# When the weights are loaded beside the tiles of attention: one by one with every third tile

## The chip, the cores and the metric

The kernel runs on one core of a Trainium2 chip. The metric is the device time of one execution in microseconds (us), as a median over several runs. It is written for the engines directly: TensorE (PE) for matmuls, VectorE (DVE), ScalarE (ACT), GpSimd (POOL), and SyncE (SP), whose queue issues all the DMAs of the kernel. The engines meet by semaphores alone.

## The reference

Three networks in a row, all in float32.

```
# attention with decay, batch 8, heads 8, sequence 576, head width 64
scores = (q @ k.T) / sqrt(64)
ret    = scores * gamma[h] ** (i - j)   where i >= j, else 0
x      = ret @ v                        # -> 4608 tokens x 512
# soft mixture of experts, 8 experts x 4 slots
logits = x @ phi                        # 4608 x 32
d = softmax over tokens(logits);  c = softmax over slots(logits)
slot_in = d.T @ x;  slot_out[e] = relu(slot_in[e] @ w1[e]) @ w2[e]
x = c @ slot_out
# product of two linear maps
h = ((x @ fw1) * (x @ fw2)) @ w3;  out = h @ w_out
```

## The kernel before

**Attention** goes over 36 tiles (NTILES, four groups of nine). A tile is 128 rows of q, k and v for all eight heads, 1 MB, and its rows are two chunks of 64 of the recurrent form of the attention. `load_tile` (L439 to L444) brings tile n into `pkg_sb`, which has four places (SLOTS_IN). From tile 4 on it first waits for `out_ready`, that is until TensorE has used tile n - 4 for the last time. The first two tiles come in two halves each (`load_first`). GpSimd scales the V of each tile by a decay (`scale_v`, L561) as soon as the tile has landed; TensorE may touch the tile's scores only after that.

On TensorE, `step` (L741 to L769) handles tile n: it begins with the scores and state updates of tile n + 1 (`scores`, L648, and `update`, L661, which wait for the scaled V), then takes the logits of tile n - 2 (L711), the part of the output that goes through the states (L676), the part through the scores, first half (L693), the transpose of tile n - 1 (`turn_x`, L705), and the second half (L693), at whose end `out_ready` is counted up. In three of the steps a `dispatch` (L727, L732) is added. The steps stand in a hardware loop over four tiles (L777 to L779, nine passes), so the instructions of the first pass are run again in the other eight. VectorE masks the scores (L1207), sums the states (L1230) and scales the output (L1249); ScalarE copies it (L1007).

**Weights.** There are 36 expert units of 1 MB (`unit_a`, `unit_x` and others: w1, w2, fw1 and fw2) and six fold parts of 1 MB (`fold_raw`: w3 twice and w_out, two parts each, called by g = 0, 1, 2 and j = 0, 1). `load_first_unit` (L452) loads the units 0 to 5, which have places of their own, during attention, with one semaphore `first_units_loaded`. `load_fold` (L446) loads the fold parts; four of them, (0, 0), (2, 0), (0, 1), (2, 1), come during attention. Every load is one `dma_start` in SyncE's program, and SyncE waits at a semaphore in its own order. So a load stands in the queue where the program puts it: unit 0 behind tile 3; the units 1 and 2 behind tile 4; 3 and 4 behind tile 5; 5 behind tile 8; the fold parts behind the tiles 10, 11, 14 and 15 (FOLD_AT). From tile 16 on only tiles are loaded.

Who uses them: ScalarE splits the fold parts into a high and a low piece (`split_hi`, L1052 to L1066), three times during attention, at the tiles 18, 22 and 26 (FOLD_HI_AT, the first four rows of j = 0 serve the first four splits), the rest behind it. GpSimd makes the low pieces (L588). The units 0 to 5 are first used by TensorE in `expert_unit` (L799), behind attention.

**Behind attention** the other units come as the buffers of attention are freed: units 6 to 8 wait for the outputs of the last tiles, the next for the buffers of others (L489 to L509). TensorE multiplies fold parts (`fold_part`, L794) between the expert units (L809). Then come the pair products (L931) and the last loop over the output (L991).

Of the kernel before, what the change touches and what calls it, by code (L numbers as in the profile page):

```python
# [48 lines left out]
FT = FF // P  # L49
EPS = 1e-9  # L50
SLOTS_IN = 4
# [1 line left out]
NAT_RING = 12  # L53
QUARTERS = 4
EARLY = 3
FOLD_AT = (10, 11, 14, 15)
FOLD_HI_AT, FOLD_LO_AT = (18, 22, 26), (21, 23, 25, 27, 29, 31)


# [21 lines left out]
def build(nc, pkg, consts, phi, units, fold_w, out, c_rows):  # L81
    ctx = ExitStack()
    with ctx:
        def sem(name):
            return ctx.enter_context(nc.semaphore(name))
# [129 lines left out]
        def unit(u):  # L215
            return {"a": unit_a, "x": unit_x, "y": unit_y, "n": unit_n, "f": unit_f}[places[u][0]][:, places[u][1], :]
# [14 lines left out]
        decay_loaded = sem("decay_loaded")  # L231
        decay_ready = sem("decay_ready")
        phi_loaded = sem("phi_loaded")
        fold_loaded = sem("fold_loaded")
        fold_late_loaded = [sem(f"fold_late_loaded{j}") for j in range(FT // 4)]
        tile_loaded = [sem(f"tile_loaded{i}") for i in range(SLOTS_IN)]
        first_loaded = [sem(f"first_loaded{i}") for i in range(2)]
# [1 line left out]
        scores_ready = [sem(f"scores_ready{i}") for i in range(2)]  # L239
# [79 lines left out]
        def fold_place(w):  # L319

            return fold_early[w - 1] if w in (1, EARLY - 1) else fold_hl[w % 2]

        def place_of(n):
            return n % SLOTS_IN

        def tile_sb(n):
            return pkg_sb[:, place_of(n), :]
# [57 lines left out]
        def chunks(engine, step):  # L385

            step(0, 0)
            with engine.Fori(0, CHUNKS // 2 - 1) as i:
                for r in range(2):
                    step(i * 2 + (r + 1), (r + 1) % 2)  # L390
            for n in (CHUNKS - 2, CHUNKS - 1):
                step(n, n % 2)
# [44 lines left out]
        @block.sync  # L437
        def _(sp):
            def load_tile(n):  # L439

                if n >= SLOTS_IN:

                    sp.wait_ge(out_ready, QUARTERS * (n - SLOTS_IN + 1))
                sp.dma_start(tile_sb(n), pkg[n].rearrange("(p c) -> p c", p=P)).then_inc(tile_loaded[place_of(n)], 16)  # L444

            def load_fold(g, j):  # L446

                sp.dma_start(fold_raw[:, g, 4 * j:4 * j + 4, :],
                             fold_w[g, j].rearrange("p (j f) -> p j f", j=4)
                             ).then_inc(fold_late_loaded[j] if g == 1 else fold_loaded, 16)  # L450

            def load_first_unit(u):  # L452

                sp.dma_start(unit_a[:, u, :], units[u].rearrange("(p c) -> p c", p=P)).then_inc(first_units_loaded, 16)

            def load_first(t, half):

                lo, hi = 2 * D * half, 2 * D * (half + 1)
                sp.dma_start(pkg_sb[:, t, lo:hi], pkg[t].rearrange("(p c) -> p c", p=P)[:, lo:hi]
                             ).then_inc(tile_loaded[t] if half else first_loaded[t], 16)  # L460

            sp.dma_start(const_sb[:, 0:C_LATE], consts[:, 0:C_LATE]).then_inc(const_loaded, 16)
            for t in range(2):
                load_first(t, 1)
                load_first(t, 0)
            sp.dma_start(x_decay[:, :, 0:P], consts[:, C_XDECAY:C_ALL].rearrange("p (a n) -> p a n", a=PAIRS)
                         ).then_inc(decay_loaded, 16)
            sp.dma_start(const_sb[:, C_LATE:C_XDECAY], consts[:, C_LATE:C_XDECAY]).then_inc(const_late_loaded, 16)
            sp.dma_start(phi_sb[:, :, :], phi).then_inc(phi_loaded, 16)
            load_tile(2)  # L470
            load_tile(3)
            load_first_unit(0)
            for n in range(SLOTS_IN, NTILES):
                load_tile(n)
                if n < SLOTS_IN + 2:
                    load_first_unit(2 * n - 7)
                    load_first_unit(2 * n - 6)
                elif n == 8:
                    load_first_unit(5)
                elif n in FOLD_AT:  # L480
                    at = FOLD_AT.index(n)
                    load_fold(at // 2 * 2, at % 2)

            def load_unit(u):


                sp.dma_start(unit(u), units[u].rearrange("(p c) -> p c", p=P)).then_inc(unit_loaded[places[u]], 16)

            for u in range(6, UNITS):  # L489
                if 6 <= u < 9:  # L490

                    sp.wait_ge(out_ready, QUARTERS * (NTILES - 3 + (u - 6)))
                if u == 9:

                    sp.wait_ge(x_turned, NTILES)
                if u == 11:

                    sp.wait_ge(sums_ready, SUBS * GROUPS)
                if places[u] == ("f", 0) and earlier[u] is None:

                    sp.wait_ge(fold_used, FT)
                if earlier[u] is not None:

                    sp.wait_ge(unit_used, earlier[u] + 1)
                load_unit(u)
                if u in (12, 14):

                    sp.wait_ge(fold_used, EARLY)
                    load_fold(1, u // 2 - 6)  # L509

            sp.wait_ge(c_t_ready, len(C_TURNS))
            for q in range(4):
                for lo, n in ((0, SLOTS), (SLOTS, ROWS - SLOTS)):
                    sp.dma_start(c_rows[lo:lo + n, :].rearrange("s (m q t) -> q s m t", q=4, t=P)[q],
                                 c_t[SLOTS * q:SLOTS * q + n, :, :]).then_inc(c_stored, 16)

            def load_c(n, s):

                base = c_rows[:, bass.ds(n * (CHUNK * P), CHUNK * P)]
                for a, (at, step) in enumerate(C_SHIFTS):  # L520
                    src = bass.AP(base.tensor, base.offset + at * TOKENS,
                                  [[TOKENS, SLOTS], [step * TOKENS, 4], [1, CHUNK * P]])
                    sp.dma_start(c_sb[:, s, a, :], src).then_inc(c_loaded[s], 16)
                src = bass.AP(base.tensor, base.offset, [[0, 4], [TOKENS, SLOTS], [1, CHUNK * P]])
                sp.dma_start(c_sb[:, s, 4, :], src).then_inc(c_loaded[s], 16)


            sp.wait_ge(unit_used, UNITS)
            sp.wait_ge(c_stored, 16 * 8)
            load_c(0, 0)  # L530
            load_c(1, 1)

            def chunk(n, s):
                if not (isinstance(n, int) and n >= CHUNKS - 2):

                    made = (n + 1) * 5
                    sp.wait_ge(feat_ready, made if isinstance(n, int) else sp.snap(made))
                    load_c(n + 2, s)
                for b in range(CHUNK):

                    copied, tile = n * CHUNK + (b + 1), n * CHUNK + b
                    if not isinstance(n, int):
                        copied, tile = sp.snap(copied), sp.snap(tile)
                    sp.wait_ge(final_copied, copied)
                    sp.dma_start(out[bass.ds(tile, 1)].rearrange("n p c -> (n p) c"),
                                 out_sb[:, b, :]).then_inc(stored[b], 16)

            chunks(sp, chunk)
            for b in range(CHUNK):
                sp.wait_ge(stored[b], 16 * CHUNKS)  # L550
# [451 lines left out]
        def _(act):  # L1002
# [49 lines left out]
            def split_hi(w):  # L1052

                half, j = divmod(w, FT)
                if w == 0:
                    act.wait_ge(fold_loaded, 16 * 4)
                if w >= FT and w % 4 == 0:
                    act.wait_ge(fold_late_loaded[(w - FT) // 4], 16)
                if w == EARLY:

                    act.wait_ge(out_ready, QUARTERS * NTILES)
                    act.wait_ge(logits_ready, SUBS * NTILES)
                if w > EARLY:
                    act.wait_ge(fold_used, 1 if w == EARLY + 1 else w - 1)
                copy(fold_place(w)["w3_hi"][:, :], fold_raw[:, half, j, :]).then_inc(fold_hi, 1)
                copy(fold_place(w)["wo_hi"][:, :], fold_raw[:, 2, j, :]).then_inc(fold_hi, 1)  # L1066
# [21 lines left out]
            for n in range(1, NTILES):  # L1088
                g, t = divmod(n, TILES)
# [12 lines left out]
                if n in FOLD_HI_AT:  # L1102
                    split_hi(FOLD_HI_AT.index(n))

            g = GROUPS - 1
# [5 lines left out]
            nc.scalar.activation(weight[:, :], neg_max[:, :], ACT.Exp, bias=neg_all[:, :],  # L1111
                                 scale=-1.0).then_inc(weight_ready, 1)
            split_hi(3)
            exp_combine(g)
            for w in range(4, 2 * FT):
# [461 lines left out]
```

## Time and profile before

| what | us |
|---|---|
| median of the three timed runs | 393.11 (389.04 to 394.10) |
| the profiled execution | 394.4 |
| span of its trace | 392.6 |
| TensorE busy (matmuls) | 358.9, 91% |
| VectorE, ScalarE, GpSimd busy | 167.5, 125.2, 161.9 |
| DMA of the kernel | 104.77 MB, mean 267 GB/s |

The span is the time from the first to the last instruction in the trace; the timed figure holds a little more around it. Matmuls are pipelined and their ends are modelled. "Issue" as the reason of an idle gap means that the engine waited for nothing that the profile can show. The granted clock of TensorE is given as a share of its full 2.4 GHz.

### The profile page before, as it was taken

To read this page: it belongs to the slowest core of one execution; us is meant where nothing else is said; L and a number is where in the kernel's file an instruction comes from. 1 tells how busy PE (TensorE), PEld (TensorE's weight loads), DVE (VectorE), ACT (ScalarE), POOL (GpSimd) and SP (SyncE) were. 2 spreads that over 40 slices of the span, in tenths; PEclk is the share of its full clock that TensorE was granted. 3 is DMA by queue.
4 is the path that set the end of the run, shared out by engine and by line. 5 is a ranking of instruction groups with operands and counts; after the bars stand their busy time and mean duration, and the time that the engine had idled before them with its cause. 6 is when DMAs were issued, how large, how long until landed. Compare 5 with 4: busy or idle time off the path is not lost. (4 is left out here: it accounts for less than half of the span.)

```text
span 392.6 us, 16090 instructions
## 1 busy us (share of the span) xinstructions
PE 358.9 (91%) x7123; PEld 278.2 (71%) x7123; DVE 167.5 (43%) x329; ACT 125.2 (32%) x275; POOL 161.9 (41%) x155
## 2 busy tenths in 40 slices
PE   2683987898999999999999999899999999999996
PEld 1573876777878887774656555468878888888885
DVE  1321454556757765573013000699853323233320
ACT  1000121321433342222324220532734444434442
POOL 2521222322443542133546451298954554554530
PEclk9856799999999999999999999999999999999999
DMA  7898499897887886879999996057226655556222
GB/s 262 351 387 341 149 398 426 337 374 250 312 308 240 313 310 231 314 294 411 427 425 427 425 428 273 0 92 237 76 88 228 230 189 188 190 179 235 114 107 107
DMA packets 25914, 104.77 MB, mean 267 GB/s; under 512 B 2660, under 2 KB 5284, under 8 KB 16164
## 3 DMA queue, kind: packets, MB, share of 16 engines
q1 hardware_dynamic: 25892, 104.47, 71.1%
q8 instruction: 14, 0.23, 0.2%
q14 instruction: 8, 0.07, 0.0%
HBM read 94.14 MB, written 10.32 MB: 266 GB/s over the span
## 5 line engine op out<-in xcount | busy, mean ns | idle before, releaser
L561 POOL TENSOR_TENSOR pkg_sb<-pkg_sb,const_sb 128x512 f32<-128x512 f32 x36 | 37.5, 1042 | 106.4 <-DMA pkg_sb<-in_tiles 106.4
L623 POOL TENSOR_TENSOR feat<-c_sb 128x512 f32<-128x512 f32 x45 | 56.9, 1275 | 46.2 <-PE psum L991 44.3
L991 PE MATMUL psum<-m_hi,feat_hi 128*128 128x512 f32 x144 | 56.1, 390 | 0.3 <-DVE m_lo L1480 0.3
L991 PE MATMUL psum<-m_lo,feat_hi 128*128 128x512 f32 x144 | 56.0, 389 | 0.0
L991 PE MATMUL psum<-m_hi,feat_lo 128*128 128x512 f32 x144 | 56.0, 389 | 0.0
L428 DVE TENSOR_TENSOR feat_lo<-feat,feat_hi 128x512 fp32r<-128x512 f32 x34 | 27.2, 801 | 62.2 <-ACT feat_hi L1149 61.0
L1249 DVE TENSOR_TENSOR x_t<-psum,x_decay 128x512 f32<-128x512 f32 x36 | 24.9, 691 | 40.9 <-PE psum L693 40.9
L1007 ACT COPY x_nat<-psum 128x512 f32<-128x512 f32 x36 | 21.1, 586 | 65.8 <-PE psum L705 65.8
L648 PE MATMUL psum<-pkg_sb 64*64 64x64 f32 x1152 | 26.9, 234 | 16.2 <-POOL pkg_sb L561 7.3
L693 PE MATMUL psum<-weights_t,pkg_sb 64*64 64x64 f32 x1152 | 35.3, 238 | 5.7 <-issue 5.5
L1149 ACT CAST feat_hi<-feat 128x512 fp32r<-128x512 f32 x45 | 27.9, 623 | 39.0 <-POOL feat L623 39.0
L588 POOL TENSOR_TENSOR w_lo<-fold_raw,w_hi 128x512 fp32r<-128x512 f32 x14 | 18.2, 1298 | 45.1 <-ACT wo_hi L1066 45.0
L648 PEld LDWEIGHTS psum<-pkg_sb 64*64 64x64 f32 x1152 | 23.4, 146 | 17.7 <-issue 17.5
L693 PEld LDWEIGHTS psum<-weights_t,pkg_sb 64*64 64x64 f32 x1152 | 26.2, 141 | 12.9 <-issue 12.6
L991 PEld LDWEIGHTS psum<-m_hi,feat_hi 128*128 128x128 f32 x144 | 27.0, 188 | 6.2 <-issue 0.7
L1207 DVE TENSOR_TENSOR weights_t<-psum,const_sb 128x512 f32<-128x512 f32 x36 | 24.7, 686 | 15.6 <-PE psum L648 14.9
L991 PEld LDWEIGHTS psum<-m_hi,feat_lo 128*128 128x128 f32 x144 | 27.0, 188 | 5.6
L991 PEld LDWEIGHTS psum<-m_lo,feat_hi 128*128 128x128 f32 x144 | 27.0, 188 | 5.6
L1230 DVE TENSOR_TENSOR state_sb<-psum,state_sb 128x256 f32<-128x256 f32 x56 | 23.5, 420 | 14.7 <-PE psum L676 12.4
L676 PE MATMUL psum<-pkg_sb,state_sb 64*64 64x64 f32 x1152 | 26.7, 234 | 2.1 <-issue 1.6
L1193 ACT COPY out_sb<-psum 128x512 f32<-128x512 f32 x36 | 21.2, 589 | 21.5 <-PE psum L991 19.5
L661 PE MATMUL psum<-pkg_sb 64*64 64x64 f32 x1152 | 27.3, 234 | 0.7 <-issue 0.7
(138 smaller groups left out, 569.0 us busy)
## 6 DMA issues: line engine op xcount, KB each, us to landing
pkg_sb<-in_tiles SPq DMA_DIRECT2D x34, 1024.0 KB, 4.9
unit_a<-in_units SPq DMA_DIRECT2D x16, 1024.0 KB, 13.8
c_sb<-c_rows SPq DMA_DIRECT2D x45, 256.0 KB
unit_x<-in_units SPq DMA_DIRECT2D x9, 1024.0 KB, 14.1
out<-out_sb SPq DMA_DIRECT2D x36, 256.0 KB, 2.0
fold_raw<-in_fold SPq DMA_DIRECT2D x6, 1024.0 KB, 9.3
unit_y<-in_units SPq DMA_DIRECT2D x5, 1024.0 KB, 12.3
unit_n<-in_units SPq DMA_DIRECT2D x4, 1024.0 KB, 12.2
```

Of the source, the lines that this page charges most:

```text
L428: engine.tensor_tensor(feat_lo[:, k, :], feat[:, k, :], feat_hi[:, k, :].bitcast(F32), ALU.subtract).then_inc(done, 1)
L561: nc.gpsimd.tensor_tensor(v_nat(n).rearrange("p (h d) -> p h d", h=HEADS), v_nat(n).rearrange("p (h d) -> p h d", h=HEADS), decay.unsqueez ...
L623: nc.gpsimd.tensor_tensor(feat[:, k, :], c_sb[:, s, x, :], c_sb[:, s, y, :], ALU.mult).then_inc(feat_ready, 1)
L648: last = mm(psum[cols, odd, HD * a:HD * (a + 1)], k_t(r)[rows, a, cols], q_t(r)[rows, a, cols], start=True, stop=True)
L661: last = mm(psum[HD * odd:HD * (odd + 1), UPDATE + half, HD * a:HD * (a + 1)], k_nat(r)[rows, cols], v_nat(r)[rows, cols], start=True, sto ...
L676: last = mm(out_of(a, odd, half), state_sb[rows, (2 * r + half) % STATES_IN, a, :], q_t(r)[rows, a, HD * half:HD * (half + 1)], start=(hal ...
L693: last = mm(out_of(a, odd, half), v_nat(r)[rows, HD * h:HD * (h + 1)], weights_t[rows, r % 2, odd, HD * a:HD * (a + 1)], start=False, stop ...
L991: last = mm(psum[:, OUT + b, :], x, y, start=(at == 0 and m == 0), stop=(at == 4 and m == 2))
L1149: copy(feat_hi[:, ORDER[at], :], feat[:, ORDER[at], :]).then_inc(feat_hi_ready, 1)
L1207: tt(weights_t[:, n % 2, :, :].rearrange("p k (a n) -> p k a n", a=PAIRS), psum[:, 0:2, 0:D // 2].rearrange("p k (a n) -> p k a n", a=PAIR ...
L1230: tt(to, new, state_sb[:, c % STATES_IN, :, :].rearrange("p a n -> p (a n)"), ALU.add).then_inc(done, 1)
L1249: tt(x_t[:, n % 2, :, :].rearrange("p (k b) n -> p k (b n)", k=2), psum[:, OUT_T:OUT_T + 2, 0:D // 2], x_decay[:, :, n0:n0 + P].rearrange( ...
```

## The change

Only the place of loads in SyncE's program is changed, and what waits for the fold parts. SyncE waits for the scores of tile 1 (`scores_ready[0]`, counted up twice per tile) before it issues unit 0. The nine other weights stand in a list and are issued one by one, behind the tiles 4, 7, 10, 13, 16, 19, 22, 25 and 28: fold parts (0, 0) and (2, 0), units 1 to 5, fold parts (0, 1) and (2, 1). The fold parts of j = 0 and of j = 1 get a semaphore each, and ScalarE waits for the first before its first split and for the second before its fifth.

```diff
-FOLD_AT = (10, 11, 14, 15)
+FIRST_WEIGHTS = 1
...
-        fold_loaded = sem("fold_loaded")
+        fold_loaded = [sem(f"fold_loaded{j}") for j in range(FT // 4)]
...
-                             ).then_inc(fold_late_loaded[j] if g == 1 else fold_loaded, 16)
+                             ).then_inc(fold_late_loaded[j] if g == 1 else fold_loaded[j], 16)
...
-            for t in range(2):
-                load_first(t, 1)
-                load_first(t, 0)
+            load_first(0, 1)
+            load_first(0, 0)
+            load_first(1, 1)
+            load_first(1, 0)
...
             load_tile(2)
             load_tile(3)
+            sp.wait_ge(scores_ready[0], 4)
             load_first_unit(0)
+            weights = ([(load_fold, g, 0) for g in (0, 2)] + [(load_first_unit, u) for u in range(FIRST_WEIGHTS, 6)]
+                       + [(load_fold, g, 1) for g in (0, 2)])
             for n in range(SLOTS_IN, NTILES):
                 load_tile(n)
-                if n < SLOTS_IN + 2:
-                    load_first_unit(2 * n - 7)
-                    load_first_unit(2 * n - 6)
-                elif n == 8:
-                    load_first_unit(5)
-                elif n in FOLD_AT:
-                    at = FOLD_AT.index(n)
-                    load_fold(at // 2 * 2, at % 2)
+                if n % 3 == 1 and n // 3 <= len(weights):
+                    load, *which = weights[n // 3 - 1]
+                    load(*which)
...
-                if w == 0:
-                    act.wait_ge(fold_loaded, 16 * 4)
+                if w in (0, 4):
+                    act.wait_ge(fold_loaded[w // 4], 16 * 2)
```

## Rows read from the trace of the kernel before

**Rows 1.** The page: span, TensorE busy, and clock and GB/s in 40 slices.
```profile
span 392.6 us, 16090 instructions
...
PE 358.9 (91%) x7123; PEld 278.2 (71%) x7123; DVE 167.5 (43%) x329; ACT 125.2 (32%) x275; POOL 161.9 (41%) x155
...
PEclk9856799999999999999999999999999999999999
...
GB/s 262 351 387 341 149 398 426 337 374 250 312 308 240 313 310 231 314 294 411 427 425 427 425 428 273 0 92 237 76 88 228 230 189 188 190 179 235 114 107 107
```

**Rows 2.** Stretches: start:end, length, busy time of each engine, PEclk, DMA share, GB/s.
```profile
30.70:34.00 3.30, 1.06 (x57) 1.03 (x60) 0.57 (x1) 0.00 (x0) 1.04 (x1) 0.97 0.99 412
34.10:44.20 10.10, 6.71 (x209) 5.76 (x207) 2.83 (x7) 0.77 (x2) 1.04 (x1) 0.51 0.48 162
...
52.80:103.50 50.70, 43.17 (x2004) 36.81 (x2000) 28.66 (x58) 12.21 (x38) 12.51 (x12) 1.00 0.90 346
103.50:158.90 55.40, 54.85 (x2526) 46.38 (x2522) 36.64 (x76) 20.09 (x62) 23.07 (x21) 1.00 0.81 284
...
172.00:244.00 72.00, 72.00 (x478) 41.83 (x467) 12.24 (x22) 18.62 (x34) 32.81 (x26) 1.00 0.97 407
```

**Rows 3.** TensorE's timeline: start, busy, operation, count [idle before it <-releaser].
```profile
10.12 1.13 PE L648 MATMUL psum<-pkg_sb 64*64 64x64 f32 x32 [1.48 <-DVE state_sb L1230]
...
16.93 0.58 PE L693 MATMUL psum<-weights_t,pkg_sb 64*64 64x64 f32 x10 [2.98 <-issue]
...
26.30 0.58 PE L661 MATMUL psum<-pkg_sb 64*64 64x64 f32 x10 [0.72 <-issue]
...
32.94 0.34 PE L693 MATMUL psum<-weights_t,pkg_sb 64*64 64x64 f32 x8 [2.52 <-issue]
...
38.68 0.31 PE L711 MATMUL psum<-x_t,phi_sb 128*32 128x32 f32 x2 [3.39 <-issue]
38.92 1.13 PE L676 MATMUL psum<-pkg_sb,state_sb 64*64 64x64 f32 x32
...
42.07 1.13 PE L648 MATMUL psum<-pkg_sb 64*64 64x64 f32 x32
...
44.39 0.69 PE L676 MATMUL psum<-pkg_sb,state_sb 64*64 64x64 f32 x32
...
46.21 0.68 PE L648 MATMUL psum<-pkg_sb 64*64 64x64 f32 x32
...
52.85 0.68 PE L648 MATMUL psum<-pkg_sb 64*64 64x64 f32 x32
```

**Rows 4.** Instruction queue in three windows: 30.7 to 30.9, 36.3 to 36.5, 40.0 to 40.2.
```profile
q8 instruction: 1, 0.02, 30.3%
...
q8 instruction: 1, 0.02, 29.9%
...
q8 instruction: 1, 0.02, 32.3%
```

**Rows 5.** SyncE's timeline from 24.6 us, and the landing of the second unit.
```profile
24.61 1.05 SPq L454 DMA_DIRECT2D unit_a<-in_units  x2
...
DMA to landing us min/median/max: 11.9/11.9/11.9
```

**Rows 6.** TensorE's waits from 46 to 103 us (total, times, longest); TensorE's and GpSimd's timelines.
```profile
PE psum L648 <- POOL pkg_sb L561: 7.3, 6, 1.5
...
57.48 0.69 PE L648 MATMUL psum<-pkg_sb 64*64 64x64 f32 x32 [1.17 <-POOL pkg_sb L561]
...
31.20 1.04 POOL L561 TENSOR_TENSOR pkg_sb<-pkg_sb,const_sb 128x512 f32<-128x512 f32 x1 [6.47 <-DMA pkg_sb<-in_tiles]
```

**Rows 7.** Landings of L444: tile issued at 49.9, at 53.2, and all from 103 us.
```profile
DMA to landing us min/median/max: 6.3/6.3/6.3
...
DMA to landing us min/median/max: 7.9/7.9/7.9
...
DMA to landing us min/median/max: 4.6/4.8/4.9
```

## The prediction

> **What bounds the kernel now.** I read the page's head and its clock row first [rows 1]: one core, TensorE busy in 91% of 392.6 us, and its granted clock low only near the start. So time can be saved where TensorE waits or runs at half clock, and where the order of loads decides that. The table of stretches comes next [rows 2]. Attention ends near 163 us, and it has three parts. Up to 44.2 us the clock lies often at its lower level (0.51 from 34.1 on, that is 1.2 GHz; the clock digits of the page show it from about 17 us). From 52.8 to 103.5 us the DMA engines are 0.90 busy and TensorE only 43.17 of 50.70 us. From 103.5 to 158.9 us only tiles are loaded, and TensorE is busy in 54.85 of 55.40 us. Behind attention, from 172 to 244 us, DMA moves at a share of 0.97: that part is a stream of expert weights that starts when attention lets go of its buffers, so it shifts with the end of attention and is not made shorter or longer by it.
>
> In the first part the timeline of TensorE shows idle gaps put down to "issue": 2.98, 1.63, 0.72, 2.52 and 3.39 us, 11.2 in all [rows 3]. What they wait for can be seen from the DMA kinds: 2.1 to 2.3 us before the ends of the last two gaps one packet of 16 KB (0.02 MB) starts on the instruction queue [rows 4], at 30.7 to 30.9 for the end at 32.94, and at 36.3 to 36.5 for the end at 38.68. These are the pieces of the loop over four tiles (L777), loaded in its first pass; one more starts at 40.0 to 40.2, and TensorE shows no such gap in any later tile of attention. How long a load takes to start depends on what is queued. Counted from the moment TensorE took up the piece before it: 26.30 to 30.8, 4.5 us; 32.94 to 36.4, 3.5 us; 38.68 to 40.1, 1.4 us. In the first two cases expert units were in the queue: two were issued from 24.61 on, the second of which landed 11.9 us after its issue at 25.2, so at 37.1 [rows 5]. In the third they were gone.
>
> In the second part TensorE waits for V to be scaled, which waits for its tile: six waits, 7.3 us [rows 6], nearly all of the 7.5 (50.70 - 43.17) that it idles there. A tile alone in the queue lands 4.6 to 4.9 us after its issue (14 of 14 after 103 us). The tile behind unit 5, issued at 49.9, took 6.3 us, and the next, at 53.2, took 7.9 [rows 7].
>
> **The change part by part.** Up to 26 us I expect almost the same course. Unit 0 now goes out right behind tile 3; it will go out when the scores of tile 1 are done, near 11.3 us (10.12 + 1.13 [rows 3]). Tile 3 is still on its way then, so the unit keeps its place in the queue. The wait stands on SyncE; behind it stands only tile 4, and that waits for the output of tile 0, which comes after the gap that ends at 16.93, in any case. Cost: 0. The first two gaps stay (tiles 2 and 3 are in front of the first load, and the second comes when the queue is nearly empty), and the third, 0.72, I leave too: tile 4 and one weight, now a fold weight in place of unit 1, are in front of it, and that is as much as it waited for.
>
> Then three units fall out of the queue (2, 3 and 4). Tile 5 has been issued at 24.24 and is alone: 4.7 us later, at 28.9, it has landed. A piece of code requested at 26.3 starts by then at the latest and is there 2.0 us later, at 30.7 to 30.9. TensorE reaches the place at 30.42. The gap of 2.52 becomes 0.3: 2.2 gained. The next request falls near 30.7 into an empty queue: start after 1.4, ready 2.1 later, at 34.2. TensorE needs 2.4 us for this piece at full clock (32.94 to 35.29), from 30.7 to 33.1. The gap of 3.39 becomes about 1.2: 2.2 gained. With gaps of 0.3 and 1.2 in place of 2.5 and 3.4 the clock need not fall: today it rises at 30.7 after a stretch without a long gap and falls at 34.1 after the gap of 2.52, while in the second part gaps of 1.2 to 1.5 us per tile leave it at 1.00 [rows 2, 6]. The lower clock from 34.1 to 44.2 costs, by the same work at both levels [rows 3]: from the states' matmul to the next scores 3.15 us (38.92 to 42.07) against 1.82 (44.39 to 46.21), so 1.3; and the tile from 42.07 to 46.21, 4.14 against 3.32 for a free tile of the second part (6.64 for two, 46.21 to 52.85), so 0.8. Early gain: 2.2 + 2.2 + 1.3 + 0.8 = 6.5. Tile 5 costs nothing on the way: its V was ready from 32.2 on [rows 6], and its scores came at 42.07 (36 to 37 after the change).
>
> The waits of the second part, 7.5, go with the pairs of weights that made them. In their place comes one weight behind each of the tiles 7, 10, 13 and so on to 28: eight (the one behind tile 4 is in the part above). Each hits the tile behind it. The model is tile 9, behind unit 5: issued at 49.9, landed at 56.2, its scores at 57.48 after a wait of 1.17. So TensorE wanted it at 56.31, 6.4 us after its issue, and 1.3 of these go to GpSimd's product and the hand-over: 5.1 are left for the transfer. Alone it needs 4.7 and is in time; behind a weight it needs 6.3 and is 1.2 late [rows 6, 7]. Over all five weights of the second part (unit 5 and four folds) the mean is 7.5 / 5 = 1.5. Lower bound for one weight: 0.4, if its transfer only fills what TensorE leaves: four transfers of 2.46 us (1.05 MB at the 427 GB/s of the busiest slices of [rows 1]) are 9.8 us, and three free tiles take 10.0 (3 x 3.32). Upper bound: one whole transfer, 2.5, if an engine stays behind. I take 1.35, between the single case and the mean: 8 x 1.35 = 10.8.
>
> Other edits: each fold semaphore now counts two loads, and ScalarE waits for the second pair at its fifth split, behind attention. The first pair lands with tile 7, long before tile 18 where it is used; the second with tile 28, some 25 us before its use. Unit 5, the last of the six for the first expert product, comes with tile 22, over 60 us before it. Price 0; if that cover were gone a late unit would cost its 4.7 us once.
>
> Sum: 392.6 - 6.5 - 7.5 + 10.8 = 389.4 us of span. The profiled execution took 394.4, 1.8 more than its span, so 391.2 for such a one; it lay 1.3 above the median of the three. Against the median: 393.1 - 3.2 = 389.9. Much of what is won early is given back in equal slices later.
>
> A rule of the Trainium skill bears on the code loads: "Runtime: NRT & Kernel Launch", Instruction fetch mechanics, says that an engine fetches its code ahead in blocks of 16 KiB and that crossing a block is mostly hidden. The trace has the blocks, and has them hidden nowhere in the first pass where the queue is full (3.39 us bare). By the page the early term would be 0.
>
> **The rivals.** A: the weights hide nearly whole, 0.4 each, 3.2 in all. For it: the transfers of three tiles and a weight fit into TensorE's time for three tiles. Against it: the one clean case cost 1.17. Time: 393.1 - 6.5 - 7.5 + 3.2 = 382.3.
>
> B, slower: one of the 16 DMA engines falls behind by a transfer and does not recover, since at 9.8 of 10.0 us there is no slack. Tile 10 took 7.9 us, 1.6 more than tile 9, though no weight stood between them. If every weight drags that along, it costs 2.5: 20.0 in all, and 393.1 - 14.0 + 20.0 = 399.1. It decides from (6.5 + 7.5) / 8 = 1.75 us a weight on. Against it: after 100 us tiles landed in 4.6 to 4.9 again.
>
> C: the code loads come no earlier. They may be bound by their own way, and the clock may fall all the same. Then the early term is near 0 and the result 393.1 - 7.5 + 10.8 = 396.4. Against it: 4.5 and 3.5 us with a full queue, 1.4 with an empty one. The skill has a ground for it beside the one above: by "DMA: Bandwidth & Descriptors", Queues, rings and completion order, an engine takes turns between its queues packet by packet, so a code load would not wait for whole transfers queued in another one. The trace speaks rather against that, with its 4.5 us.
>
> **How the numbers follow.** Forecast 0.54, A 0.17, B 0.13, C 0.16. A measurement of this kernel tells about 2% (7.9 us) from no change: below 385.2 is faster, above 401.0 slower. Faster: all but a little of A and some of the forecast's tail (price 0.75 or less), 0.20. Slower: the upper end of B, 0.05. Same: 0.75. The forecast's own range is 386 to 394 (price 0.85 to 1.85). The range for 8 in 10 reaches into both other sides: 383.5 to 397.
>
> **What would show it.** Right: the gaps of "issue" before 45 us sum to 6 to 8 us in place of 11.2; the clock stays at 1.00 from about 31 us; scores of tile 8 begin near 47 to 48 in place of 52.85; then TensorE waits for V of the tiles 8, 11, 14 and so on, about 1.2 us each and eight of them, also past 103 us where no wait is now; those tiles land after 6 to 6.5 us, the others after 4.7 to 5.5; the expert part is as long as before. Wrong: gaps as long as today's (C); two or three waits per weight (B); waits of under half a microsecond (A); or the expert stream longer than now.

## The result, and the profile after the change

The changed kernel is slower: 396.51 us (median of four runs, 394.95 to 397.22) against 393.06 for the kernel before in the same runs (389.04 to 394.10). The ratio is 1.0115, with a 95% interval of 1.0062 to 1.0167. That lies in my range (383.5 to 397), but I had forecast 389.9, on the other side of the kernel before. It is a difference under 2%, so the verdict is "same" by that measure, but it is clear of the noise.

The profiled execution took 396.42 us. The page's head and its rows in 40 slices, the answer to [rows 1]:

```profile
span 394.6 us, 16091 instructions
...
PE 357.3 (91%) x7123; PEld 276.5 (70%) x7123; DVE 167.7 (42%) x329; ACT 125.2 (32%) x275; POOL 161.7 (41%) x155
...
PEclk9978999999999989999999999999999999999999
...
GB/s 259 360 291 119 392 363 342 339 323 355 336 305 296 355 228 257 299 290 411 430 423 426 427 425 318 1 90 231 54 115 233 218 177 198 184 188 235 113 106 106
```

The clock row is higher at the start than before, and it has a dip at slice 15 that was not there. The stretches, in the columns of [rows 2]:

```profile
30.70:34.00 3.30, 1.52 (x98) 1.34 (x94) 1.62 (x3) 0.00 (x0) 1.04 (x1) 1.00 0.58 216
34.10:44.20 10.10, 9.41 (x380) 8.26 (x381) 4.60 (x9) 1.73 (x5) 2.08 (x2) 0.83 0.55 218
52.80:103.50 50.70, 44.41 (x2068) 37.96 (x2072) 29.43 (x61) 14.01 (x45) 13.73 (x13) 1.00 0.94 343
103.50:161.20 57.70, 51.90 (x2280) 43.55 (x2282) 33.91 (x70) 17.16 (x52) 20.78 (x19) 0.97 0.79 291
141.30:144.60 3.30, 3.30 (x127) 3.02 (x121) 1.59 (x4) 0.19 (x1) 2.27 (x2) 0.53 0.66 266
174.30:246.30 72.00, 72.00 (x479) 41.83 (x467) 12.24 (x22) 18.61 (x34) 32.80 (x26) 1.00 0.97 407
```

From 34.1 to 44.2 us TensorE now works 9.41 us in place of 6.71, and the clock is 0.83 in place of 0.51. Past 103.5 us it is idle for 5.8 us (57.70 - 51.90) where it was idle for 0.6, and around 143 us the clock is at its lower level. The expert part in the last row is the same to the digit of its PE time and its GB/s.

TensorE's timeline, the rows that answer to [rows 3], and some of the late scores (those of the tiles 22, 23, 29, 30, 31 and 35):

```profile
16.77 0.39 PE L692 MATMUL psum<-weights_t,pkg_sb 64*64 64x64 f32 x10 [2.02 <-issue]
...
20.53 1.13 PE L675 MATMUL psum<-pkg_sb,state_sb 64*64 64x64 f32 x32 [2.44 <-issue]
...
26.39 0.39 PE L660 MATMUL psum<-pkg_sb 64*64 64x64 f32 x10 [1.23 <-issue]
...
30.41 0.34 PE L692 MATMUL psum<-weights_t,pkg_sb 64*64 64x64 f32 x8 [1.32 <-issue]
...
34.78 0.25 PE L710 MATMUL psum<-x_t,phi_sb 128*32 128x32 f32 x2 [2.56 <-issue]
34.96 0.99 PE L675 MATMUL psum<-pkg_sb,state_sb 64*64 64x64 f32 x32
...
37.97 0.96 PE L647 MATMUL psum<-pkg_sb 64*64 64x64 f32 x32
...
44.88 0.68 PE L647 MATMUL psum<-pkg_sb 64*64 64x64 f32 x32
...
106.63 0.69 PE L647 MATMUL psum<-pkg_sb 64*64 64x64 f32 x32 [0.86 <-POOL pkg_sb L560]
...
112.11 0.59 PE L647 MATMUL psum<-pkg_sb 64*64 64x64 f32 x25 [1.94 <-POOL pkg_sb L560]
...
135.68 0.69 PE L647 MATMUL psum<-pkg_sb 64*64 64x64 f32 x32 [1.11 <-POOL pkg_sb L560]
...
140.71 0.94 PE L647 MATMUL psum<-pkg_sb 64*64 64x64 f32 x32 [1.55 <-POOL pkg_sb L560]
...
145.36 0.68 PE L647 MATMUL psum<-pkg_sb 64*64 64x64 f32 x32
...
161.21 0.68 PE L647 MATMUL psum<-pkg_sb 64*64 64x64 f32 x32
```

The scores of tile 5 start at 37.97 (42.07 before), those of tile 7 at 44.88 (49.57 before): 4.7 us gained. At tile 35 they start at 161.21, and before at 158.89, so 2.3 us are lost:

```profile
158.89 0.68 PE L648 MATMUL psum<-pkg_sb 64*64 64x64 f32 x32
```

So between the tiles 7 and 35 the change loses 7.0 us, and from tile 35 on both kernels take the same to the end of the span, 233.7 us before and 233.4 after. TensorE's waits in two windows, from 46 to 103 us and from 103 to 160 us (total, times, longest), answer to [rows 6]:

```profile
PE psum L647 <- POOL pkg_sb L560: 6.8, 7, 1.5
...
PE psum L647 <- POOL pkg_sb L560: 5.5, 4, 1.9
```

Eleven waits and 12.3 us stand against six and 7.3.

### The profile page after: what moved, and what is told of

It is laid out like the page before. It is cut to its first block and busy times, and to the rows that moved or that the text cites. A ratio compares the mean times of both kernels' runs of the same rounds, so it can differ in the third digit from the quotient of the medians.

```text
span 394.6 us, 16091 instructions
## 1 busy us (share of the span) xinstructions
PE 357.3 (91%) x7123; PEld 276.5 (70%) x7123; DVE 167.7 (42%) x329; ACT 125.2 (32%) x275; POOL 161.7 (41%) x155
## 5 line engine op out<-in xcount | busy, mean ns | idle before, releaser
L647 PE MATMUL psum<-pkg_sb 64*64 64x64 f32 x1152 | 26.6, 233 | 21.8 <-POOL pkg_sb L560 12.3
L587 POOL TENSOR_TENSOR w_lo<-fold_raw,w_hi 128x512 fp32r<-128x512 f32 x14 | 18.2, 1297 | 45.3 <-ACT wo_hi L1065 45.1
L692 PEld LDWEIGHTS psum<-weights_t,pkg_sb 64*64 64x64 f32 x1152 | 26.0, 141 | 10.6 <-issue 10.3
L660 PE MATMUL psum<-pkg_sb 64*64 64x64 f32 x1152 | 26.2, 228 | 1.2 <-issue 1.2
## 6 DMA issues: line engine op xcount, KB each, us to landing
unit_y<-in_units SPq DMA_DIRECT2D x5, 1024.0 KB, 12.2
```

The lines of the kernel that those rows point to most:

```text
L647: last = mm(psum[cols, odd, HD * a:HD * (a + 1)], k_t(r)[rows, a, cols], q_t(r)[rows, a, cols], start=True, stop=True)
L660: last = mm(psum[HD * odd:HD * (odd + 1), UPDATE + half, HD * a:HD * (a + 1)], k_nat(r)[rows, cols], v_nat(r)[rows, cols], start=True, sto ...
L692: last = mm(out_of(a, odd, half), v_nat(r)[rows, HD * h:HD * (h + 1)], weights_t[rows, r % 2, odd, HD * a:HD * (a + 1)], start=False, stop ...
```

## The experiments

One number serves for all of them: the time from the scores of tile 7 to those of tile 35, less 101.6 us. The 101.6 is what two of the runs below give for these 28 steps without their one wait for V (102.81 - 1.16 and 102.93 - 1.35). What is left is what the weights behind the tiles from 7 on cost, waits and clock together. The columns "tile 7" and "tile 35" give the start of the tile's first `scores` matmul in TensorE's timeline; "waits" is the sum of the waits for V from 46 us on; "cost, each" is that cost and its share per weight. Each row is one profile.

| kernel | tile 7 | tile 35 | waits | weights from tile 7 on | cost, each |
|---|---|---|---|---|---|
| before | 49.57 | 158.89 | 7.3 | 5 | 7.7, 1.5 |
| before, second profile | 48.20 | 157.26 | 7.0 | 5 | 7.5, 1.5 |
| changed | 44.88 | 161.21 | 12.3 | 8 | 14.7, 1.8 |
| changed, second profile | 46.27 | 159.73 | 9.9 | 8 | 11.9, 1.5 |
| changed, no wait for unit 0 | 45.74 | 160.64 | 9.7 | 8 | 13.3, 1.7 |
| every fourth tile | 44.91 | 157.58 | 9.0 | 7 | 11.1, 1.6 |
| every sixth tile | 44.88 | 151.63 | 4.3 | 5 | 5.2, 1.0 |
| pairs | 45.15 | 164.59 | 12.2 | 8 | 17.8, 2.2 |
| early part only | 45.04 | 156.32 | 9.1 | 8 | 9.7, 1.2 |
| later part only | 50.02 | 160.09 | 5.7 | 5 | 8.5, 1.7 |
| after the tiles | 43.93 | 146.74 | 1.2 | 1 | 1.2 |
| five behind | 45.34 | 148.27 | 1.4 | 3 | 1.3, 0.4 |

**The two parts apart.** The later part alone keeps the pairs behind the tiles 4 and 5 and spaces the rest:

```diff
-            weights = ([(load_fold, g, 0) for g in (0, 2)] + [(load_first_unit, u) for u in range(FIRST_WEIGHTS, 6)]
-                       + [(load_fold, g, 1) for g in (0, 2)])
+            at = {4: [(load_first_unit, 1), (load_first_unit, 2)], 5: [(load_first_unit, 3), (load_first_unit, 4)],
+                  7: [(load_fold, 0, 0)], 10: [(load_fold, 2, 0)], 13: [(load_first_unit, 5)],
+                  16: [(load_fold, 0, 1)], 19: [(load_fold, 2, 1)]}
...
```

> The later part of the change alone: the units 1 to 4 in pairs behind tiles 4 and 5 as before, but then unit 5 and the four folds singly behind every third tile (7, 10, 13, 16, 19) in place of 8, 10, 11, 14, 15. If a single weight at every third tile costs 1.5 to 1.8 us: scores of tile 7 at 49 to 50 us as before, waits of 7.5 to 9 us over the five, tile 35 at 158.5 to 160, time 393 to 395, no gain from spacing them. If spacing pays, the waits are under 6 us and the time 389 to 391.

Measured: 394.22 us (median of ten), ratio 1.0026 (0.9995 to 1.0057). Only three waits, but long ones (1.99 at tile 8, 2.01 at tile 12, 1.65 at tile 17), 5.7 us in all; with what follows them the five weights cost 8.5. The waits are under 6 us, as the branch in which spacing pays had it, but the time is that of the other branch: spacing them by three tiles gains nothing over the order 8, 10, 11, 14, 15. The early part alone:

```diff
+            late = {4: (load_first_unit, 1), 8: (load_first_unit, 5), 10: (load_fold, 0, 0), 11: (load_fold, 2, 0),
+                    14: (load_fold, 0, 1), 15: (load_fold, 2, 1), 18: (load_first_unit, 2),
+                    22: (load_first_unit, 3), 26: (load_first_unit, 4)}
...
```

> The early part of the change alone: unit 0 after the scores of tile 1, one weight behind tile 4, none behind tile 5; from tile 8 on the order of the kernel before (unit 5 at 8, folds at 10, 11, 14, 15), and the units 2, 3 and 4 singly behind 18, 22 and 26. Theory 1: scores of tile 7 near 45 us as in the changed kernel (49.6 before); the waits of tiles 9 to 17 about 7.5 us as before; three singles at 1.2 to 1.7 each, 4 to 5 us; tile 35 at 158 to 159; time 391 to 394. Theory 2 (the early gain is lost again later since the tiles come when they come): tile 17 at 93 as before and the singles on top, tile 35 at 162 or more.

Measured: 393.26 us (ten runs), ratio 0.9994 (0.9949 to 1.0039). Tile 7 at 45.04 as expected, and the single weights behind 18, 22 and 26 gave waits of 0.74, 1.11, 1.82 and 0.61. The three units that left the early tiles gave 4.5 us there and took about as much back at their new places. So neither part alone moves the time clear of the noise.

**How a weight's price depends on the spacing.** Every sixth tile, the rest behind tile 35:

```diff
-                if n % 3 == 1 and n // 3 <= len(weights):
+                if n in (4, 7, 13, 19, 25, 31):
+                    load, *which = weights[(4, 7, 13, 19, 25, 31).index(n)]
...
+            for load, *which in weights[6:]:
+                load(*which)
```

> The changed kernel, but from tile 7 on only every sixth tile has a weight behind it (7, 13, 19, 25, 31); unit 5 and the fold parts of j = 1 go out behind tile 35. Five single weights with time to recover between them. If a weight by itself costs 1.7 us (two late tiles), the waits for V sum to 8 to 9 us over the five. If the second late tile comes only because weights at every third tile leave the DMA engines no slack, it is 1.2 each, 5 to 6 us, and the tiles two behind a weight show no wait.

Measured: 386.85 us in one run (the kernel before: 393.9 in the runs beside it). Five waits, 4.3 us, less than either branch had, and only one of them (0.25 at tile 10) is not right behind a weight. The landings of the tiles 13 to 17 there, the weight standing between 13 and 14:

```profile
DMA to landing us min/median/max: 4.6/4.6/4.6
...
DMA to landing us min/median/max: 6.3/6.3/6.3
...
DMA to landing us min/median/max: 7.1/7.1/7.1
...
DMA to landing us min/median/max: 6.3/6.3/6.3
...
DMA to landing us min/median/max: 4.7/4.7/4.7
```

This is a reading that my prediction lacked. One weight makes not one tile late but three: 6.3, 7.1 and 6.3 us, and only the fourth lands after 4.7 again. But the three late landings bring only one wait here, 0.81 us at tile 14. With a weight behind every third tile the next one comes just when the landings are in time again, and they stay late. That shows in the landings of all tiles issued from 46 to 150 us, first in the changed kernel (25 tiles), then in the kernel below that issues no weight from 46 us until all tiles are issued (26 tiles):

```profile
DMA to landing us min/median/max: 4.7/7.1/8.5
```

```profile
DMA to landing us min/median/max: 4.7/4.8/4.9
```

Every fourth tile:

```diff
-                if n % 3 == 1 and n // 3 <= len(weights):
-                    load, *which = weights[n // 3 - 1]
+                if n == 4 or n % 4 == 3:
+                    load, *which = weights[0 if n == 4 else n // 4]
```

> The changed kernel with a weight behind every fourth tile from 7 on (7, 11, to 31, and the last behind 35): seven of the eight stay among the tiles, with one tile more between them to catch up. Price by the number of weights (1.5 to 1.7 each): waits of 10.5 to 12 us. Price by spacing (0.9 each at every sixth tile, 1.7 at every third): 1.1 to 1.3 each, 8 to 9 us, tile 35 near 155 to 157, whole time 389 to 392.

Measured: 392.81 us in one run (before: 391.24). 9.0 us of waits, just above what the price by spacing said, but 11.1 us of cost, 1.6 each: 1.7 of the rest is one step at a lower clock (below), 7.45 us from the scores of tile 32 on in place of 5.76. The spacing does not tell the whole price. Two of the seven weights, behind the tiles 15 and 23, brought no wait; behind 11, 19 and 27 it was 1.7 to 2.1 us each. A weight behind tile 19 brought 1.9 us of waits here and 1.0 at every sixth tile, though in both runs the tiles before it had landed in time (4.7 or 4.8 us).

The same eight in pairs behind 7, 13, 19 and 25:

```diff
+                at = [weights[0:1], weights[1:3], weights[3:5], weights[5:7], weights[7:9]]
+                if n in (4, 7, 13, 19, 25):
...
```

> The same nine weights in attention as in the changed kernel, but from tile 7 on in pairs behind every sixth tile (7, 13, 19, 25). If what costs is that four transfers for three tiles leave the DMA engines no time to catch up, the mean load is the same and so are the waits, 11 to 14 us. If each weight has a price of its own (1.5), 12. If a pair makes one long delay and then recovers for four tiles, the first tile behind is late by 3.6 and the second by about 1: 4.5 a pair, 18 in all.

Measured: 399.81 us in one run (before: 391.24), waits of 3.32, 3.15, 3.46 and 2.06 us, and steps up to 2.8 us longer behind the first three of them. With a small one of 0.16 they sum to 12.2. The branch of the mean load (11 to 14) and that of a price of its own for each weight (12) both said so, and this run can't tell them apart. Three of the first waits are near the 3.6 of the third branch, but its wait at the second tile is missing. The cost is the highest of all, 17.8.

**The clock.** Why cost and waits differ is seen in the run of the later part alone. TensorE's timeline around its first wait, and the stretches before, of and behind the step that follows:

```profile
55.47 1.09 PE L647 MATMUL psum<-pkg_sb 64*64 64x64 f32 x32 [1.99 <-POOL pkg_sb L560]
...
60.42 0.69 PE L647 MATMUL psum<-pkg_sb 64*64 64x64 f32 x32
...
63.72 0.68 PE L647 MATMUL psum<-pkg_sb 64*64 64x64 f32 x32
```

```profile
51.90:55.40 3.50, 1.58 (x56) 1.21 (x48) 1.24 (x3) 0.59 (x1) 1.04 (x1) 1.00 0.97 328
55.50:60.40 4.90, 4.79 (x164) 4.24 (x165) 1.29 (x3) 0.65 (x2) 1.04 (x1) 0.65 0.96 390
60.40:63.70 3.30, 3.28 (x164) 2.96 (x168) 2.14 (x4) 0.47 (x3) 1.04 (x1) 1.00 0.67 226
```

Behind the wait of 1.99 us the granted clock is 0.65 on average, TensorE is busy nearly all the time, and the step takes 4.95 us; the same step takes 3.61 in the run "five behind", where the clock is 1.00. So a wait of two microseconds costs 3.3. In the changed kernel the same happens once, at tile 30: the wait of 1.55 ending at 140.71, the clock 0.53 from 141.3 to 144.6, and the next step 4.65 us (to 145.36) in place of 3.35.

It does not happen behind every such wait. The longest one of the changed kernel, 1.94 us at tile 23, ends at 112.11, and the step behind it runs at full clock:

```profile
112.10:117.50 5.40, 5.39 (x184) 3.79 (x188) 1.83 (x4) 0.78 (x3) 2.14 (x2) 1.00 0.92 366
```

In the other profiles the clock fell behind waits of 1.79 (no wait for unit 0) and 1.94 us (every fourth), and stayed behind 1.82 (early part only) and 2.06 (pairs). What tells the two kinds apart no run here shows. The steps at a lower clock took 1.1 to 2.8 us longer than the same steps at the full one.

**Smaller pieces.** If a weight's 2.46 us are too long, quarters should slip through. Quarters of 32 rows, one behind each tile from 5 on:

```diff
+                sp.dma_start(unit_a[lo:hi, u, :], units[u].rearrange("(p c) -> p c", p=P)[lo:hi]
+                             ).then_inc(first_units_loaded, 16)
...
```

> The changed kernel, but the weights behind unit 0 and the first fold part go out in quarters of 256 KB, one behind each of the tiles 5 to 35 (and one more at the end). Same bytes in attention. Theory 1 (a whole weight makes the next tile late by 1.2 us and leaves one of the DMA engines behind, so that a second tile is late): a quarter takes 0.6 us and fits into the gap between the landing of one tile (4.7 us after its issue) and the first bytes of the next (3.3 + 2.2 = 5.5 us after it), so nearly no wait for V: the waits of the changed kernel between 46 and 160 us, 12.3 us, become under 3, the scores of tile 35 begin near 150 (161.2 in the changed kernel), time 384 to 388. Theory 2 (the bytes themselves cost, the DMA engines have no room beside the tiles): waits stay at 9 to 13 us, time 394 to 398.

Measured: 405.14 us (four runs, 395.7 to 409.4, a spread too wide for a ratio; the kernel before: 393.9), and in the profile, of an execution of 402.9 us, 20 waits for V, 16.3 us. In that profile the DMA engines are busy 0.97 of the time from 50 to 100 us and move 313 GB/s. That is outside both branches of what I expected. The profiled execution took 7 us more than the fastest of the same kernel, so it says little of the idea. The form of the quarter may spoil the test, so the next run takes columns of all 128 partitions:

```diff
+                sp.dma_start(unit_a[:, u, lo:hi], units[u].rearrange("(p c) -> p c", p=P)[:, lo:hi]
+                             ).then_inc(first_units_loaded, 16)
...
```

> As the run with quarters, but each quarter is 512 columns of all 128 partitions (2 KB a row) in place of 32 whole rows. If the quarters were dear because 32 rows slowed the packets down (their mean rose from 357 to 402 ns there), the packets of the tiles are back at 309 and the waits between 46 and 160 us are under 5 us, tile 35 near 152. If any traffic between two tiles makes the second late, the waits stay above 12 us and tile 35 is at 160 or later.

Measured: 391.60 us in one run (before: 391.24), waits of 6.1 us, 0.94 busy at 346 GB/s, tile 35 at 156.43. In this one run that is better than whole weights at every third tile, but it is neither branch of what I expected: a quarter is not hidden either, and three of its waits were 1.6 to 2.1 us.

**Unit 0's wait.**

```diff
-            sp.wait_ge(scores_ready[0], 4)
```

> The changed kernel without SyncE's wait for the scores of tile 1: unit 0 goes out behind tile 3 as before. By my step (its place in the queue is the same either way) nothing changes: first gap of TensorE 2.0 to 3.0 us, scores of tile 7 at 44.3 to 45.5 us, time within 2 us of the changed kernel's 396.5. If the wait matters, the first gap grows by 1 us or more.

Measured: 395.87 us in one run, first gap 2.99, tile 7 at 45.74 (44.88 and 46.27 with the wait). That is within what two profiles of one kernel differ by: no effect to be seen.

**Out of attention.** Seven weights behind tile 35, in front of the expert stream:

```diff
+                if n in (4, 7):
+                    load, *which = weights[(4, 7).index(n)]
...
+            for load, *which in weights[2:]:
+                load(*which)
```

> The changed kernel with only unit 0 and the fold parts of j = 0 in attention (behind tiles 4 and 7); the seven others go out behind tile 35. Attention without weights: no wait for V but one of 0.8 to 1.2 at tile 8, scores of tile 35 near 148 (161.2 in the changed kernel, so the seven weights' own price is 13 us). The whole kernel does not gain that, since seven transfers of 2.46 us, 17 us, stand in front of the expert stream: 395 to 402 us.

Measured: 387.58 us in one run, far below the 395 to 402 that I expected. The scores of tile 35 come 14.5 us earlier, at 146.74, and of the 17 us of transfers only 5.4 show: 239.1 us from tile 35 to the end, against 233.7 in the kernel before. With three weights there (every sixth tile) the rest took 233.4, so three are free. The stretch from 146 to 172 us shows the room, in the kernel before and in this one:

```profile
146.00:172.00 26.00, 25.29 (x897) 19.76 (x899) 15.42 (x42) 8.09 (x21) 3.76 (x4) 1.00 0.75 273
```

```profile
146.00:172.00 26.00, 25.50 (x472) 17.56 (x473) 15.49 (x40) 6.75 (x17) 5.75 (x5) 1.00 1.01 426
```

The DMA engines were busy 0.75 there and are full now. Hence a version between the two:

```diff
-                if n % 3 == 1 and n // 3 <= len(weights):
-                    load, *which = weights[n // 3 - 1]
+                if n in (4, 7, 15, 25):
+                    load, *which = weights[(4, 7, 15, 25).index(n)]
...
+            for load, *which in weights[4:]:
+                load(*which)
```

> The changed kernel with fewer weights among the tiles: fold parts of j = 0 behind tiles 4 and 7, units 1 and 2 behind 15 and 25, and the five others behind tile 35. From tile 35 on the kernel took 233.4 to 233.7 us with none and with three weights there, and 239.1 with seven, so the queue has room for some. If the price of a weight far from the next is 1.0 to 1.2 us: tile 35 at 149 to 150, the rest 234 to 236, time 384 to 387, faster than both kernels by 2%. If what was gained in the two single looks was chance (before: 389 to 394 in its own runs), the median is above 390.

Measured: 383.22 us (median of six), ratio to the kernel before 0.9731 (0.9688 to 0.9774): 2.7% faster than before. TensorE's waits from 46 to 148 us, and two stretches of attention:

```profile
PE psum L649 <- POOL pkg_sb L562: 1.4, 1, 1.4
```

```profile
46.00:103.00 57.00, 55.03 (x2605) 47.51 (x2599) 36.54 (x77) 17.76 (x57) 18.68 (x18) 1.00 0.84 313
103.00:146.00 43.00, 42.52 (x1932) 35.57 (x1932) 27.98 (x58) 14.48 (x41) 16.96 (x16) 1.00 0.82 305
```

Its one wait is behind tile 7. The scores of tile 35 begin at 148.27, and the rest takes 233.5 us, so five weights are free there. The weights behind 15 and 25 cost nothing, less than I expected. Both stand beside a step with a dispatch, which takes 5.4 us in place of 3.3 (76.06 - 70.61 for the one at tile 14): it comes before tile 16 is wanted, and between the issues of the tiles 25 and 26. That the places are cheap for this reason is my reading. The other profiles fit it: behind 15, 23 and 25 a weight brought no wait at every fourth and every sixth tile either, and at all other places from 7 on one did in those two. So the low price of this run and of every sixth tile (1.0) is partly one of the place, and no run changed the spacing without the places.

**Both kernels once more.**

> The kernel before, a second profile of it, to see how much the waits of one profile vary. The first lay 1.3 us above the median of its runs. Waits for V of 6 to 9 us (7.3 in the first), gaps of issue of 9 to 12 us before 46 us (11.2), tile 35 at 156 to 159.

> The changed kernel, a second profile. If its late waits belong to it and not to one execution: again 10 to 14 us of waits for V from 46 us on (12.3), also past 103 us, the scores of tile 7 at 44 to 46, tile 35 at 160 to 162.

Measured: 392.74 and 394.98 us. Before: gaps of issue 10.6, waits 7.0, tile 7 at 48.20 and tile 35 at 157.26, so the first profile lay 1.6 us later at tile 35. Changed: waits of 9.9 us, just under the 10 I gave as the lower end, late ones again past 103 us, tile 7 at 46.27 and tile 35 at 159.73, both just outside what I gave. The mean gain at tile 7 over two profiles each is 3.3 us (48.9 - 45.6), not the 4.7 of the first pair. Other profiles bear on it too: over all eight with one whole weight behind tile 4, none behind 5 and the wait for unit 0, tile 7 comes at 45.1 in the mean, over the three with two pairs there at 49.3, a gain of 4.2.

## Why the prediction was wrong

**Up to 26 us, right.** "Almost the same course" held: gaps of 2.02, 2.44 and 1.23 us in place of 2.98, 1.63 and 0.72, 5.7 against 5.3 in sum. Unit 0's wait costs nothing, by the run without it.

**The code loads, right in kind and near in size, but not in the gaps.** The fourth piece was to be there by 30.7 to 30.9 and the fifth at 34.2; TensorE went on at 30.41 and 34.78. Against 32.94 and 38.68 that is 3.9 us of the 4.4 forecast at this point. Rival C falls in its main part: with the units 2 to 4 out of the queue the loads do come earlier, in every one of the kernels that moved them (tile 7 at 43.9 to 46.3, against 48.2 to 50.0 in the three profiles with the old order). The gaps themselves sum to 9.6 us, and to 9.7 in the second profile, where I had asked for 6 to 8: the pieces came as early as forecast or nearly so, but TensorE reached the place sooner, at 29.09 and not at 30.42, because its clock was at 1.00 (26.39 to 29.09) and not at 0.50 as in the first profile of the kernel before (26.30 to 30.42). In the second profile of that kernel it is at 1.00 there too (26.37 to 29.07), so this is not won by the change. The Trainium skill, "Runtime: NRT & Kernel Launch", Instruction fetch mechanics, says that crossing a block is mostly hidden. In the first pass of this loop the trace does not agree: in the changed kernel 1.2 to 2.6 us still stay bare at each of the five crossings.

**The clock, the step that failed first.** I took 2.1 us (1.3 + 0.8), as "the clock need not fall" with gaps of 0.3 and 1.2 us. The gaps were 1.32 and 2.56. The fifth was longer because the piece came at 34.8 and not 34.2, and because at full clock TensorE needs only 1.81 us for the work in front of it (30.41 to 32.22); the 2.4 that I took for full clock, from 32.94 to 35.29, were at 0.69. The two stretches, before and after:

```profile
32.94:35.29 2.35, 2.35 (x102) 2.07 (x102) 1.62 (x3) 0.00 (x0) 0.00 (x0) 0.69 1.08 408
```

```profile
30.41:32.22 1.81, 1.81 (x102) 1.60 (x102) 1.32 (x2) 0.00 (x0) 1.04 (x1) 1.00 0.19 54
```

Behind the gap of 2.56 the clock fell, and in the second profile already behind the fourth gap, of 1.59 us. In the first profile it was 0.83 from 34.1 to 44.2, and it took 3.01 us from the states' matmul at 34.96 to the scores of tile 5 at 37.97, near the 3.15 of half clock and far from the 1.82 of full. From the fifth piece of code to tile 7 the change gained 0.8 us (4.7 - 3.9) and not 2.1, and in the pair of second profiles nothing (2.2 at the piece, 35.17 against 37.32, and 1.9 at tile 7). With this the early term was 4.7 in the first pair, 3.3 in the mean of both and 4.2 over the eight profiles against three, not 6.5. One step further the same belief hid a cost: behind some of the waits for V the clock falls too.

**The weights' price, mis-sized: its waits were right, and what follows a wait was put at nothing.** I set it at "1.35, between the single case and the mean: 8 x 1.35 = 10.8". The three profiles with a weight behind every third tile gave 14.7, 11.9 and 13.3 us, a mean of 1.66 each. Their waits are 12.3, 9.9 and 9.7 us, 1.33 a weight, so the waits came out at the forecast. The steps at a lower clock took 1.3, 1.4 and 2.8 us more than the same steps in "five behind", 0.23 a weight, and the other 0.10 is a little that a step with a wait takes beyond the wait. That the waits met the 1.35 is partly luck. I had taken one tile as a model ("Each hits the tile behind it") and let the tile after it go; it stood in the rows with 7.9 us beside the 6.3, and I gave that to rival B. The tiles landed after 7.1 us in the median of all 25, where I had 6 to 6.5 for those behind a weight and 4.7 to 5.5 for the others, and the waits were not eight of 1.2 us but eleven, eight and seven, of 1.1 to 1.4 us in the mean.

Rival B had the late second tile: a delay that is carried on because there is no slack. Its price was too high (2.5 each), and so was its sign, two or three waits per weight, where about one came. Its threshold of 1.75 fell when the early term shrank: with 3.3 us gained it is (3.3 + 7.6) / 8 = 1.36, and with 4.2 it is 1.48, so that a price not far above my own made the kernel slower. That a single DMA engine falls behind is not shown; the lateness is.

**The sum.** By the means: 393.1 - 3.3 - 7.6 + 13.3 = 395.5 (394.6 with an early gain of 4.2), against 396.5 measured. Forecast: -6.5, -7.5, +10.8. So the early term fell short by 2.3 to 3.2 us and the price by 2.5, and 1.0 to 1.9 us stay unexplained, about what two profiles of one kernel differ by (1.5 and 1.6 us at tile 35). The removed waits were sized right. The expert part is as long as before, and the fold and unit semaphores cost nothing, as said.

**Rival A, wrong here,** though its ground (the transfers fit by count) is true: the throughput would do, but eight weights still brought 9.7 to 12.3 us of waits. Bytes that fit on average do not keep a tile from landing late.

## What to carry to other kernels

A transfer put between others that are just in time should be priced by all the tiles that it delays, up to the one that lands on time again, and by what the waits may do to TensorE's clock. Regular spacing is no cure: here even spacing gained nothing, and the two weights that cost nothing in the fastest version stood beside a long step, though no run took place and distance apart. Look first for a stretch in which the DMA engines idle and nothing is due, even behind the stage: here five weights moved to the end of attention gave 2.7%, together with the early part of the change, where spreading them gave a loss. And when a term rests on one tile of one profile, take a second profile, or let the doubt reach the side of the forecast and not only its range.

## What the runs showed of the hardware

The granted clock fell after waits for V of 1.55 us (0.53 from 141.3 to 144.6) and 1.99 us (0.65 in the next step), and it did not after one of 1.94 us (1.00 from 112.1 to 117.5), so the length of the wait alone does not decide it. A quarter megabyte in 32 whole rows looked dearer than the same in 512 columns of all partitions: 313 GB/s at 0.97 busy against 346 at 0.94, from 50 to 100 us; but that is one profile of each, the first of an execution of 402.9 us where another took 395.7, and so not shown. A weight of 1 MB in an otherwise timely stream gave landings of 6.3, 7.1, 6.3 and then 4.7 us. And two executions of one kernel differ by 1.4 us at tile 7 alone (49.57 and 48.20), so that a single profile says little of a term of that size.
